# Attention and MLP mixer: first two head pairs scored from the turned q and k, one rope table, w_tok split in later pairs

## What is computed

```python
q_rot, k_rot = rotate(q), rotate(k)      # x1*cos - x2*sin, x1*sin + x2*cos
scores = (1/sqrt(64)) * q_rot @ k_rot.T  # (4, 8, 576, 576)
attn = softmax(scores); o = attn @ v
x = o as (4, 576, 512)
u = x + (relu(x.T @ w_tok1) @ w_tok2).T
out = u + relu(u @ w_ch1) @ w_ch2
```

## Time and profile before

| | |
|---|---|
| median of 3 runs | 668.12 us (667.87 to 669.03) |
| profiled execution | 669.35 us, of which 667.6 are the span |
| PE busy | 638.3 us, 96% of the span, 4848 matmuls |
| DVE, ACT, POOL busy | 466.3 us, 409.8 us, 252.1 us |
| DMA | 60.88 MB, mean 91 GB/s |

### The profile page before, as it was taken

One profiled execution on the slowest core, in us unless ns is written; L12 is line 12 of the kernel. 1 busy time (PEld: TensorE's weight loads), 2 busy tenths in 40 slices (PEclk: granted clock), 3 DMA queues, 4 the chain that ended last, 5 costly groups with the idle time before them and its releaser, 6 DMA issues.

```text
span 667.6 us, 13576 instructions
## 1 busy us (share of the span) xinstructions
PE 638.3 (96%) x4848; PEld 621.5 (93%) x4848; DVE 466.3 (70%) x823; ACT 409.8 (61%) x916; POOL 252.1 (38%) x250
## 2 busy tenths in 40 slices
PE   1689999999999999999999999999999999999996
PEld 1589999999999999999999999999899999999996
DVE  5789999999999999976485862238830377413584
ACT  3488888888988899976464543236532255423353
POOL 1998888888888887551800000000000000000000
PEclk9999999999999999999999999999999999999998
DMA  7565666667667764406000121000210002100001
GB/s 226 145 165 154 175 173 174 181 168 181 174 175 185 189 175 121 110 14 223 4 0 1 45 60 48 1 1 2 80 72 0 0 0 79 71 1 1 1 1 72
DMA packets 60697, 60.88 MB, mean 91 GB/s; under 512 B 18912, under 2 KB 45152, under 8 KB 60640
## 3 DMA queue, kind: packets, MB, share of 16 engines
q1 hardware_dynamic: 60640, 60.12, 33.6%
HBM read 28.64 MB, written 9.44 MB: 57 GB/s over the span
## 4 chain that ended last, share of the span: by engine, by line
PE 90%; DMA 2%; POOL 2%; DVE 2%; issue 2%; SPq 1%; ACT 1%; ACTq 0%; DVEq 0%; POOLq 0%
PE slot L539 12%; PE rest L572 11%; PE rest L549 9%; PE slot L1109 7%; PE slot L1111 7%; PE slot L1110 7%; PE rest L1111 6%; PE rest L1109 6%; PE rest L1110 6%; PE rest L583 3%; PE rest L514 2%; PE rest L559 2%; PE slot L1141 2%; PE rest L1141 2%; PE rest L219 1%
## 5 line engine op out<-in xcount | busy, mean ns | idle before, releaser
L1339 DVE TENSOR_TENSOR pieces<-h,pieces 128x288 fp32r<-128x288 f32 x168 | 75.0, 453 | 88.6 <-ACT pieces L1261 88.4
L855 DVE TENSOR_REDUCE neg_max<-slot 128x1 f32<-128x576 f32 x144 | 108.0, 750 | 7.6 <-PE slot L539 2.9
L1261 ACT ACTIVATE pieces<-h 128x288 fp32r<-128x288 f32 x168 | 74.5, 443 | 46.5 <-PE slot L1111 28.5
L863 DVE TENSOR_TENSOR pt_lo<-rest,pt_hi 128x512 fp32r<-128x512 f32 x144 | 96.0, 676 | 2.5 <-ACT pt_hi L747 1.9
L572 PE MATMUL rest<-pt_hi,v 128*128 128x256 f32 (+1 forms) x320 | 89.5, 303 | 0.0
L747 ACT ACTIVATE pt_hi<-rest 128x512 fp32r<-128x512 f32 x144 | 83.9, 595 | 5.5 <-PE rest L549 4.5
L539 PE MATMUL slot<-key,q_hi 128*128 128x288 f32 x256 | 65.0, 335 | 11.0 <-DMA q_cross<-t_hi_q 6.6
L572 PE MATMUL rest<-pt_lo,v 128*128 128x256 f32 (+1 forms) x256 | 69.8, 295 | 0.0
L740 ACT ACTIVATE prob_a<-slot,neg_max 128x576 f32<-128x576 f32 x80 | 59.4, 742 | 15.4 <-DVE neg_max L855 15.2
L572 PEld LDWEIGHTS rest<-pt_hi,v 128*128 128x128 f32 x320 | 60.4, 189 | 0.0
L1352 DVE TENSOR_TENSOR h<-h 128x288 f32<-128x288 f32 x96 | 41.6, 451 | 24.8 <-ACT h L1243 24.4
(11 more groups left out here) (185 smaller groups left out, 1853.9 us busy)
## 6 DMA issues: line engine op xcount, KB each, us to landing
key<-t_hi_k SPq DMA_DIRECT2D x32, 144.0 KB, 2.3
key<-t_lo_k SPq DMA_DIRECT2D x32, 144.0 KB, 2.5
raw_qk<-in_k_dram SPq DMA_DIRECT2D x16, 256.0 KB, 2.8
raw_qk<-in_q_dram SPq DMA_DIRECT2D x16, 256.0 KB, 2.7
q_hi<-t_hi_q SPq DMA_DIRECT2D x32, 128.0 KB, 2.4
q_cross<-t_lo_q SPq DMA_DIRECT2D x32, 128.0 KB, 2.4
q_cross<-t_hi_q SPq DMA_DIRECT2D x32, 128.0 KB, 2.4
raw_v<-in_v_dram SPq DMA_DIRECT2D x16, 256.0 KB, 3.4
```

Of the source, the lines that this page charges most:

```text
L855: dve.tensor_reduce(neg_max[p % 2][:, i:i + 1], slot[g % 2][:, :, 0:HALF], AX.XY, ALU.max, negate=True).then_inc(maxed, 1)
L863: dve.tensor_tensor(pt_lo[:, :, cols], rest[:, bank, :].rearrange("p (j n) -> p j n", j=G), f32(pt_hi[:, 0:G, cols]), ALU.subtract).then_i ...
L1261: act.activation(pieces[:, ring(m), 0, :], source[WEIGHTS[n]][:, ft, :], ACT.Copy).then_inc(piece_hi, 1)
L1339: dve.tensor_tensor(pieces[:, ring(m), 1, :], source[WEIGHTS[n]][:, ft, :], f32(pieces[:, ring(m), 0, :]), ALU.subtract).then_inc(piece_lo, 1)
```

## The change

1. Pairs 0 and 1 (`DIRECT = 2`) are not assembled. Their eight tiles of one head take three passes of 64 partitions, read straight from `t_hi` and `t_lo`: six matmuls instead of four.
2. One rope table for k and q; the scale of 1/8 is put in where q's turned tile is copied out (ACT with a scale, DVE with a scalar multiply before the subtraction).
3. w_tok1 is sent for at the end of pair 1 and w_tok2 at the end of pair 2. They are split in five pieces, in pairs 3 to 7: high parts on ACT at the head of the pair's list, low parts on POOL at the end of the pair's list. The loads of w_ch1 move from pairs 2 to 9 to pairs 4 to 11.
4. Pair 0 has its own order on PE, ACT and DVE; the loop starts with pair 1. POOL splits v of head A of pair 0 ahead of its loop.

```diff
+DIRECT = 2
...
-    return np.stack([cos * scale, sin * scale, cos, sin], axis=1).reshape(P, 4 * NG * D)
+    return np.stack(tables, axis=1).reshape(P, 2 * NG * D)
...
+    w1_cols = [slice(n * NG * TOK // 2, (n + 1) * NG * TOK // 2) for n in range(2)]
+    PIECES = ([(0, [w[:].rearrange("p t n -> p (t n)")[:, cols] for w in wt1], s0[:, cols]) for cols in w1_cols] +
+              [(1, [w[:, a, 0:MAIN].rearrange("p (t j) -> p t j", t=G) for w in wt2],
+                s1[:, a * S:a * S + MAIN].rearrange("p (j t) -> p t j", t=G)) for a in range(TT)] +
+              [(1, [w[:, :, MAIN:S] for w in wt2], s1[:, 0:TT * S].rearrange("p (a s) -> p a s", a=TT)[:, :, MAIN:S])])
...
         def assemble_q(a, p):
-            if no(p):
+            if no(p) or p < DIRECT:
                 return
...
-        for n, tables in (("k", slice(2 * NG * D, 4 * NG * D)), ("q", slice(0, 2 * NG * D))):
-            sp.dma_start(rope_sb[:].rearrange("p a t d -> p (a t d)")[:, tables], rope[:, tables]).then_inc(rope_in[n], 16)
-            load(n, 0)
-        for done, (dmas, _) in zip(w_in, chunks):
-            for dst, part in dmas:
-                sp.dma_start(dst, part).then_inc(done, 16)
+        sp.dma_start(rope_sb[:].rearrange("p a t d -> p (a t d)"), rope).then_inc(rope_in, 16)
+        load("k", 0)
+        load("q", 0)
         load_next("k", 1)
         load_next("q", 1)
-        assemble_k(0, 0)
-        assemble_q(0, 0)
-        assemble_k(1, 0)
-        assemble_q(1, 0)
...
-            if 2 <= p < 2 + 2 * CT:
-                w1.load(sp, w_ch1, (p - 2) // 2, p % 2)
+            if 1 <= p <= len(chunks):
+                for dst, part in chunks[p - 1][0]:
+                    sp.dma_start(dst, part).then_inc(w_in[p - 1], 16)
+            if 4 <= p < 4 + 2 * CT:
+                w1.load(sp, w_ch1, (p - 4) // 2, p % 2)
...
+        split_v(0, "A")
         for p in range(N + 2):
...
-            split_v(p, "A")
+            if p > 0:
+                split_v(p, "A")
+            if 3 <= p < 3 + len(PIECES):
+                weights_lo(p - 3)
...
-            if t == 0:
-                pe.wait_ge(tiles_in[a], (p + 1) * ASSEMBLED)
-            if g == 0:
+            if p < DIRECT:
+                if i == 0:
+                    pe.wait_ge(t_lo_done["k"], p + 1)
+                    pe.wait_ge(t_lo_done["q"], p + 1)
+            elif t == 0:
+                pe.wait_ge(tiles_in[a], (p + 1 - DIRECT) * ASSEMBLED)
+            if g == DIRECT * TILES:
                 pe.wait_ge(zero_halves, 4)
...
+                if p < DIRECT:
+                    b, head = p % 2, slice(a * D, (a + 1) * D)
+                    passes = ((t_hi["q"][b][head, cols], t_hi["k"][b][head, :]), (t_hi["q"][b][head, cols], t_lo["k"][b][head, :]),
+                              (t_lo["q"][b][head, cols], t_hi["k"][b][head, :]))
...
-        for p in range(N):
+        for i in range(4):
+            score(0, i)
+        transposes("k", 1, K_BANKS)
+        for i in range(4, 7):
+            score(0, i)
+        turn(0, 0, 1)
+        turn_tails(0, 0, 0)
+        score(0, 7)
+        after_lo(0, 0)
+        turn(0, 1, 1)
+        after_t_lo("k", 1)
+        transposes("q", 1, Q_BANKS)
+        score(0, 8)
+        after_tails_lo(0, 0)
+        turn(0, 2, 0)
+        after_t_lo("q", 1)
+        turn(0, 3, 3)
+
+        for p in range(1, N):
...
         t_part_hi("k", 0, 0)
         t_part_hi("q", 0, 2)
-        for c in range(len(chunks)):
-            weights_hi(c)
+        for i in range(3):
+            exponent(0, i)
+        t_part_hi("k", 1, K_BANKS)
+        for i in range(3, 7):
+            exponent(0, i)
+        turned_hi(0, 0, 1)
+        tails_hi(0, 0, 0)
+        exponent(0, 7)
+        turned_hi(0, 1, 1)
+        t_part_hi("q", 1, Q_BANKS)
+        turned_hi(0, 2, 0)
+        turned_hi(0, 3, 3)
+
+        for p in range(1, N):
+            if 3 <= p < 3 + len(PIECES):
+                weights_hi(p - 3)
             copy_o(p - 2, "B1")
             exponent(p - 1, 8)
...
-        for c in range(len(chunks)):
-            weights_lo(c)
+        for i in range(4):
+            maximum(0, i)
+        t_part_lo("k", 1, K_BANKS)
+        for i in range(4, 7):
+            maximum(0, i)
+        turned_lo(0, 0, 1)
+        maximum(0, 7)
+        tails_lo(0, 0, 0)
+        turned_lo(0, 1, 1)
+        t_part_lo("q", 1, Q_BANKS)
+        turned_lo(0, 2, 0)
+        maximum(0, 8)
```

More of the change, by code:

```diff
@@ L33 @@
 RING = 5
+SCALE = float(1.0 / np.sqrt(D))
+DIRECT = 2
 F32 = mybir.dt.float32
@@ L53, in rope_tables @@
         tables.append(laid)
-    scale = np.float32(1.0 / np.sqrt(D))
-    cos, sin = tables
-    return np.stack([cos * scale, sin * scale, cos, sin], axis=1).reshape(P, 4 * NG * D)
+    return np.stack(tables, axis=1).reshape(P, 2 * NG * D)
 def f32(ap):
@@ L85, in build @@
             raw_qk = sb(placed, "raw_qk", [P, 2, 2, NG, D])
-            rope_sb = sb(placed, "rope_sb", [P, 4, NG, D])
+            rope_sb = sb(placed, "rope_sb", [P, 2, NG, D])
         pieces = sb(whole, "pieces", [P, RING, 2, HALF], F32R)
@@ L274, in attention @@
     stage = [stage_or_x[:, n * CH:(n + 1) * CH] for n in range(2)]
-    rope_in = {n: sem(f"rope_in_{n}") for n in "kq"}
+    rope_in = sem("rope_in")
     raw_in = {n: sem(f"raw_in_{n}") for n in "kqv"}
@@ L311, in rotate @@
         m, half = 2 * p + "kq".index(n), D // 2
-        cos, sin = (rope_sb[:, i].unsqueeze(1).broadcast_to([P, 2, NG, D])
-                    for i in ((0, 1) if n == "q" else (2, 3)))
+        cos, sin = (rope_sb[:, i].unsqueeze(1).broadcast_to([P, 2, NG, D]) for i in range(2))
         x = raw[n]
@@ L333, in attention @@
           (s0[0:TAIL, G * TOK:NG * TOK], w_tok1[MAIN:S]),
[L334 to L340, removed]
-    ]
+          (s0[TAIL:P, G * TOK:NG * TOK], w_tok1[MAIN:S])],),
+        ([(s1[:, 0:TT * S].rearrange("p (a s) -> p a s", a=TT), w_tok2.rearrange("(a p) s -> p a s", p=P))],),
+    ]
+    w1_cols = [slice(n * NG * TOK // 2, (n + 1) * NG * TOK // 2) for n in range(2)]
[3 more added lines that the diff above has]
+              [(1, [w[:, :, MAIN:S] for w in wt2], s1[:, 0:TT * S].rearrange("p (a s) -> p a s", a=TT)[:, :, MAIN:S])])
     def sync(sp):
@@ L428, in sync @@
             assemble_q(1, p + 1)
-            if 2 <= p < 2 + 2 * CT:
-                w1.load(sp, w_ch1, (p - 2) // 2, p % 2)
+            if 1 <= p <= len(chunks):
[3 more added lines that the diff above has]
+                w1.load(sp, w_ch1, (p - 4) // 2, p % 2)
             if p == 10:
                 sp.wait_ge(x_stored, STORED * HP)
-                sp.wait_ge(w_lo_done, len(chunks))
+                sp.wait_ge(w_lo_done, len(PIECES))
                 token.load_x(sp, 0, range(0, 2), ())
@@ L486, in normalise, with weights_lo @@
                                sums.unsqueeze(2).broadcast_to([P, NG, D]), ALU.mult).then_inc(x_done, 1)
+        def weights_lo(n):
+            _, (hi, lo), whole = PIECES[n]
+            pool.wait_ge(w_hi_done, n + 1)
+            pool.tensor_tensor(lo, whole, f32(hi), ALU.subtract).then_inc(w_lo_done, 1)
         rotate(pool, "k", 1)
         rotate(pool, "q", 1)
+        split_v(0, "A")
         for p in range(N + 2):
@@ L627, in tensor @@
             after_lo(p - 1, 5)
-            if p == 0:
-                after_t_lo("q", 0)
             transposes("k", p + 1, K_BANKS)
@@ L632, in tensor @@
             turn(p - 1, 6, 0)
-            if p > 0:
-                after_t_lo("q", p)
-                after_t_lo("k", p)
+            after_t_lo("q", p)
+            after_t_lo("k", p)
             score(p, 4)
@@ L726, in t_part_hi @@
             act.wait_ge(t_ready[n], p + 1)
-            if p >= 2:
+            if p >= DIRECT + 2:
                 for a in range(2):
-                    act.wait_ge(tiles_in[a], (p - 1) * ASSEMBLED)
-            act.activation(t_hi[n][p % 2][:], columns(bank, WIDE[n]), ACT.Copy).then_inc(t_hi_done[n], 1)
+                    act.wait_ge(tiles_in[a], (p - 1 - DIRECT) * ASSEMBLED)
+            act.activation(t_hi[n][p % 2][:], columns(bank, WIDE[n]), ACT.Copy,
+                           scale=SCALE if n == "q" else 1.0).then_inc(t_hi_done[n], 1)
         def exponent(p, i):
@@ L765, in copy_o, with weights_hi @@
             act.activation(ot[f[0]][:, to:to + n1 - n0], rest[:, PV_BANK[f], 0:n1 - n0], ACT.Copy).then_inc(ot_done[f], 1)
-        def weights_hi(c):
+        def weights_hi(n):
+            c, (hi, _), whole = PIECES[n]
             act.wait_ge(w_in[c], 16 * len(chunks[c][0]))
-            for (hi, _), part in chunks[c][1]:
-                ins = act.activation(hi, part, ACT.Copy)
-            ins.then_inc(w_hi_done, 1)
+            act.activation(hi, whole, ACT.Copy).then_inc(w_hi_done, 1)
         t_part_hi("k", 0, 0)
         t_part_hi("q", 0, 2)
-        for c in range(len(chunks)):
-            weights_hi(c)
-        for p in range(N):
+        for i in range(3):
[13 more added lines that the diff above has]
```

(21 more changed lines are left out.)

## The result

The changed kernel takes 677.43 us (median of 4) against 668.17 us: ratio 1.0138, interval 1.0117 to 1.0158, 9.3 us slower. The forecast was 667.1 us.

A forecast was written before the change was run, and what follows sets the result against it. PE alone was taken to bound the middle pairs, so an earlier start shortens the whole: 3.7 gained - 1.6 for passes - 1.05 for w_tok = 1.05 us faster, 668.12 to 667.1 us; range 665.2 to 669.1.

The forecast's parts named there:

- The start: Pairs 0 and 1: pair 1's tile 2 starts at 34.2 instead of 38.09; 3.7 us gained after 0.2 off.
- the gain of 1.05 us on q's DMA: At the start, DVE's 1.05 us idle wait for q's DMA goes away, putting the first score at 12.9.
- the prediction's faster case: In pair 0, the clock rises already for tile 2; pair 1's tile 2 then starts at 33.6.
- The extra passes: Six tiles of pair 1 have two more matmuls each, at 0.26 us per tile: 1.6 us lost.
- w_tok: Pairs 3 to 7: ACT's pieces stall PE by twice 0.07 and twice 0.45, 1.05 us lost; POOL's cost 0.
- the row with the other shape does not bear it out: On the array-drain rule: the tails' 64-column turns show no gap, so shape changes were left out of the forecast.
- The rival: Pairs 0 and 1: switching between 64 and 128 partitions empties PE, 0.16 us a change; 669.7 us, chance 0.12.
- from there with fast matmuls: Pair 0 from exponent 3, at 21.15: matmuls run at the 2.4 GHz level, making the round 1.09 + 0.78 + 0.89.
- PE having been fed for 3 us: Early in the earlier kernel, the clock rose between 22.63 and 26 us, after some 3 us with little idle.
- The chance for slower: Whole kernel slower by over 0.2%, above 669.5 us: half of the two slower cases and a bit, 0.13.
- stalls in pairs 5 and 6: Sign for w_tok on ACT: 0.45 us more in pairs 5 and 6; no stall there would break the term.
- at most 22 us between the first score and pair 1's tile 2: Sign for the start: more than 22 us between these two would break a term.

The follow-up runs named there:

- run 5: Changed kernel with pair 0's direct tiles at 128 partitions and pair 1's at 64: 668.84 us, ratio 1.0010.
- run 9: The changed kernel again, unaltered, nine executions: three from 669.6 to 670.8, six from 676.8 to 678.8; median 676.94 us, ratio 1.0097.
- run 6: Changed kernel with pair 0's direct tiles at 64 partitions and pair 1's at 128: median 668.87 us, in two groups.
- run 10: Changed kernel with full-height filler transposes on PE ahead of and around pair 0's first transposes: median 668.45 us, ratio 1.0024.
- run 4: Kernel before with only the w_tok part of the change (part 3), pairs 0 and 1 assembled as before: 666.66 us, ratio 0.9977.
- run 2: Kernel before with one head's tiles of pairs 8 and 9 scored in three passes of 64 partitions: 677.57 us, ratio 1.0139.
- run 12: Changed kernel with DIRECT = 1, pair 0 direct at 64 partitions and pair 1 assembled by DMA: 672.05 us, ratio 1.0051.

## Why the prediction was wrong

- **The start.** The mechanism held. Run 1, the changed kernel without its half height, has pair 1's tile 2 at 34.52, where 34.2 was worked out, and behind pair 1 PE waits for neither POOL nor a DMA. That the two times are so near is partly luck: the gain of 1.05 us on q's DMA was 0.24 there (q's rotation starts at 8.23 instead of 8.47, because k's starts 0.7 us later), so the first score came at 13.85 and not 12.9; and the clock rose already for tile 2, the prediction's faster case, which made up most of it.
- **The extra passes.** 0.80 per tile against 0.53, as taken, and the same six matmuls in the middle 0.115 us each (3.7 us for 32).
- **w_tok.** 1.3 us against 1.05: the long pieces stalled PE by 0.57 rather than 0.45.
- With these three, run 1's 667.14 us is near the forecast's 667.1. **The step that failed is the one that gave the 64-partition passes no price of their own**: "the row with the other shape does not bear it out". The tails' turns are 64 columns wide, and that change is free; a change in the number of partitions is not. The Trainium skill, "TensorEngine Tiling (Array Packing)", Key Properties, says that changing mode drains the array. For partitions the runs agree, at 0.17 us a change; for the 64 columns of the tails' turns they show no gap. The rival had the price right, 0.16, but a chance of only 0.12. It would have given 669.7, near run 5 and near three of the changed kernel's executions in run 9 (669.6 to 670.8).
- **The larger part, some 7 us (the distance between run 9's two groups), had no rival at all**: "from there with fast matmuls" took for granted that the clock rises as it had with full-height passes. The text spoke of PE having been fed for 3 us; it did not ask whether a half-height pass feeds it as much. The runs answer that: run 1's clock is up at 18 us, that of the same 24 matmuls at 64 partitions is not at 20. Runs 1, 5, 6, 9 and 10 together show that two things must meet for the 9 us: pair 0's stream of 64-partition passes leaves the clock at half, and pair 1's then keep it there until 46 to 49 us. Take either pair to full height and the 9 us shrink to 4 or less; bring the clock up first and 7 of 11 executions are at 668.
- The chance for slower was 0.13, the range ended at 669.1. Of the signs that the prediction named, stalls in pairs 5 and 6 showed as forecast and the first score came at 13.34, not 12.9. Two signs of a broken term showed too: 26 us instead of at most 22 between the first score and pair 1's tile 2, and gaps at the 64-partition tiles.
- What stays open: why the clock stays at half or falls back in one execution and is up in another of the same kernel. In the first 24 matmuls it is the half height that counts, since no change of height lies among them. For pair 1 it was not tried whether the gaps of the changes or the half height keep the clock down; run 1 only shows that plain idle time of that size does not.

## What to carry to other kernels

A pass over 64 partitions is not half a pass: beside its own columns it costs 0.17 us at every change to and from full height, and near the start of a kernel it may leave PE at half clock, here until 46 to 49 us. A way round a DMA is worth only what the later chain doesn't take back: the first score came 2.9 us earlier than in run 4, and pair 1 half a microsecond. Deferred work should go where the engine's row shows an idle gap, not to the head of its list: the same five pieces cost 1.3 us in one place and nothing in the other.

## What the runs showed of the hardware

- Turns with 64 columns beside full ones: no gap; scores with 64 partitions beside full ones: 0.18 us in, 0.15 out, at full clock (run 2).
- From the first score on, 24 matmuls of 128 partitions had the clock up at 18 to 19 us (runs 1 and 5); the same 24 with 64 partitions had it still at half at 20 us (changed kernel, runs 6, 9 and 12).
- At full clock a saturated stream of mixed heights keeps it: run 2 for 44 us, run 5 for one pair (by its profile, and by the times of its ten executions, which lie within 1.6 us). At half clock the same mix ran for 23 us in the changed kernel, with PE busy throughout, before it rose.
- The clock column is 1.00 before the first rise, also where the matmuls go at 1.2 GHz. The changed kernel in run 9, profiled at 676.94 us, has 1.00 here while 41 matmuls fill 10 us; a stretch at full clock has 70 to 84:

```profile
30.00:40.00 10.00, 10.00 (x41) 8.45 (x40) 5.66 (x9) 5.85 (x12) 6.01 (x7) 1.00 0.28 64
```
